# A gated recurrence and two feed-forward stages on one core: the first three levels of the recurrence's pair products in two bursts per block

## The chip, the cores and the metric

The kernel runs on one core of a Trainium2 chip. The metric is device time in microseconds (us) of one execution, as the median of the runs.

## The reference

Three layers in fp32 follow each other. Cut to what matters:

```python
# r, k, v, w: (4, 8, 768, 48)   u: (8, 48)
for t in range(768):
    cur = einsum('bhd,bhe->bhde', u * k[t], v[t])
    y[t] = einsum('bhd,bhde->bhe', r[t], state + cur)
    state = w[t][..., None] * state + einsum('bhd,bhe->bhde', k[t], v[t])
x = y.transpose(0, 2, 1, 3).reshape(3072, 384)
xn = x / sqrt(mean(x * x) + 1e-6) * rms_g
x1 = (silu(xn @ w_gate) * (xn @ w_val)) @ w_out        # 384 -> 1536 -> 384
h = relu(x1 @ w_in)
out = (s * h * h + b) @ w_out2                          # 384 -> 2048 -> 384
```

## The kernel before

**The work.** 3072 tokens are cut into six groups of 512, and each group into two blocks of two chunks of 128 tokens. The attention of group s (called stage s here, s = 0 to 5) is computed while the gated layer of group s-1 runs; the squared layer of all groups follows at the end. A stage of the gated layer has 36 steps k: gate tile, value tile and output tile in turn, each nine wide matmuls (128x128 weights, 512 moving columns; weights and x are each split in an upper and a lower part, three products for one). Between the steps every engine has a fixed list of attention work, in `attention(s, k)` of each engine. The order on an engine is the program's; engines meet by semaphores alone.

**The attention.** The recurrence with its decays is worked out by levels. K and R hold keys and queries by channel (48 channels of a head in 64 rows, two heads on 128 partitions, 8 times 128 tokens in the columns). At level l, tokens stand in runs of 2^l; the products of the first runs' keys with the second runs' queries are what that level gives. After a level the keys of first runs are multiplied by the decay over the second run (VectorE, `multiply_keys`), the queries of second runs by the decay over the first (GpSimd, `multiply_queries`), and the decays themselves are doubled (VectorE, `double_decay`, called by `decays_after`). The products of a level are matmuls of 64 rows, 64 key columns, and 32 moving query columns, 32 of them a block (8 column blocks, two halves, two heads): `level`. They land in `level_ps` (two PSUM banks, shared by both blocks: 16 tiles of 64 columns); VectorE copies what the mask of the level lets through into `near` (`place`, copy_predicated). Level 5 (`NEAR`) is copied by ScalarE (`place_near`), and level 6 by `place_far`.

**Where it is put in.** In a later stage (s > 0) levels 1 to 5 are at steps `LEVEL_AT = (3, 6, 9, 12, 15)`, both blocks in one burst of TensorE, the top level at 18. The keys are turned at 20 (chunks 0 to 2) and 22 (chunk 3), copied by ScalarE (`keys_out`), and multiplied with the values at 22 (`update` 0, 1) and 24 (`update` 2, 3); `attend` follows at 24 and 26. `advance_state` on VectorE adds the updates. At step 34 GpSimd multiplies the next stage's queries for level 0, and VectorE its decays and keys; ScalarE makes x_hi at 33.

**The gated layer on the other engines.** ScalarE makes the silu of the gate tile behind the gate step (L806) and u_hi behind the value step (`upper`, L813); VectorE the product u (`product`, L1057) in the value step and u_lo (`lower`, L1065) in the step after that. TensorE's output tile needs u_lo of its f, its next gate tile the silu, and its next value tile the product. In stage 1 ScalarE and VectorE also split weights (`upper_weights` L785, `upper_out_weights` L790; `lower_weights` L1042, `lower_out_weights` L1047), which the gated layer of the first group needs in turn.

TensorE's waits in a level are these (in the functions below `wait(pe, sem, n)` holds the engine until the count is reached):

```python
elif l > 1:
    level_out(pe, s, l - 1, blk)      # the level before has been placed
if s > 0 and l == 1:
    wait(pe, yo_done, CH * s)
keys_ready(pe, s, l, blk)
queries_ready(pe, s, l, blk)
```

## Time and profile before

| what | value |
|---|---|
| median of 3 runs | 1009.8 us (1008.68 to 1010.35) |
| the profiled execution, its own time | 1010.07 us |
| its span, first to last instruction | 1007.9 us |
| TensorE busy | 990.4 us (98%) |
| VectorE busy | 548.2 us (54%) |
| ScalarE busy | 314.0 us (31%) |
| GpSimd busy | 267.3 us (27%) |
| mean granted TensorE clock | 0.986 of full |

The rows call the engines PE (TensorE's matmuls), PEld (its weight loads), DVE (VectorE), ACT (ScalarE) and POOL (GpSimd). Matmuls overlap, so the distance between starts is what one costs, not its duration. An fp32 matmul of the program is two rows in the trace, of weights and of matmul alike. A bracket at the end of a row is the idle time of the engine ahead of it and what ended it.

### The profile page before, as it was taken

The numbers are of one execution on the slowest core, as the hardware profiler recorded it, in microseconds if no ns is written. First come the engines' busy times: TensorE is split into PE (matmuls) and PEld (weight loads), VectorE is DVE, ScalarE is ACT, GpSimd is POOL, SyncE is SP. The second block draws the span as 40 slices with busy tenths as digits, with TensorE's granted clock in tenths as the row PEclk, the third lists the DMA queues.
The fourth block names the chain that finished last, engine by engine and source line by source line (L and its number), as shares of the span: only waits on it lengthen the run. The fifth ranks groups of instructions, "written<-read, shape, count | busy, mean of one in ns | idle before, by whom it ended". The sixth has DMA issues, their size and how long they took to land.

```text
span 1007.9 us, 24185 instructions
## 1 busy us (share of the span) xinstructions
PE 990.4 (98%) x10344; PEld 830.3 (82%) x10344; DVE 548.2 (54%) x738; ACT 314.0 (31%) x530; POOL 267.3 (27%) x189
## 2 busy tenths in 40 slices
PE   7889999999999999999999999999999999999998
PEld 6778888888888888888888888888888888888898
DVE  6789866764776477557753225506337054162440
ACT  1442323232223313231323445405225043151340
POOL 4655723552464156216610560000000000000000
PEclk7799999999999999999999999999999999999999
DMA  7380252117013601440116201011020110201000
GB/s 272 119 318 15 90 158 101 49 45 224 33 49 106 194 3 49 142 158 2 49 49 207 94 28 64 1 24 40 11 52 0 21 42 10 52 0 21 11 8 24
DMA packets 70780, 74.02 MB, mean 73 GB/s; under 512 B 50464, under 2 KB 55072, under 8 KB 69408
## 3 DMA queue, kind: packets, MB, share of 16 engines
q1 hardware_dynamic: 70112, 71.52, 22.3%
q8 instruction: 75, 1.23, 0.5%
q10 hardware_dynamic: 576, 1.13, 0.3%
q14 instruction: 17, 0.14, 0.0%
HBM read 59.27 MB, written 13.37 MB: 72 GB/s over the span
## 4 chain that ended last, share of the span: by engine, by line
PE 87%; DVE 1%; issue 0%; ACT 0%; DVEq 0%
PE value_o_ps L609 13%; PE mix_gate_ps L609 13%; PE o_ps L1402 11%; PE level_ps L47 10%; PE o_ps L621 9%; PE mix_gate_ps L1402 5%; PE value_o_ps L47 5%; PE mix_gate_ps L47 5%; PE value_o_ps L621 4%; PE level_ps L481 4%; PE o_ps L1415 2%; PE mix_gate_ps L557 2%; PE level_ps L557 2%; PE mix_gate_ps L1415 1%; PE value_o_ps L1415 1%; PE level_ps L535 1%
## 5 line engine op out<-in xcount | busy, mean ns | idle before, releaser
L1189 POOL TENSOR_TENSOR R<-R,arena 128x512 f32<-128x512 f32 x72 | 117.2, 1644 | 187.6 <-PE level_ps L481 169.1
L1501 DVE SCALAR_TENSOR_TENSOR sqr<-relu,sb_col 128x512 f32<-128x512 f32 x96 | 72.3, 753 | 73.1 <-ACT relu L1463 73.1
L1057 DVE TENSOR_TENSOR u_raw<-value_o_ps,u_raw 128x512 f32<-128x512 f32 x66 | 45.5, 690 | 111.6 <-PE value_o_ps L609 111.5
L806 ACT ACTIVATE u_raw<-mix_gate_ps 128x512 f32<-128x512 f32 x72 | 43.0, 598 | 181.1 <-PE mix_gate_ps L609 181.1
L813 ACT ACTIVATE u_hi<-u_raw 128x512 fp32r<-128x512 f32 x66 | 41.7, 632 | 151.3 <-DVE u_raw L1057 151.3
L609 PE MATMUL mix_gate_ps<-x_hi,w_hi 128*128 128x512 f32 x216 | 84.8, 393 | 0.7 <-DVE x_lo L1018 0.7
L609 PE MATMUL value_o_ps<-x_hi,w_hi 128*128 128x512 f32 x216 | 85.2, 394 | 0.0
L609 PE MATMUL value_o_ps<-x_hi,w_lo 128*128 128x512 f32 x216 | 84.2, 390 | 0.0
L609 PE MATMUL value_o_ps<-x_lo,w_hi 128*128 128x512 f32 x216 | 84.2, 390 | 0.0
L609 PE MATMUL mix_gate_ps<-x_lo,w_hi 128*128 128x512 f32 x216 | 84.2, 390 | 0.0
L609 PE MATMUL mix_gate_ps<-x_hi,w_lo 128*128 128x512 f32 x216 | 84.2, 390 | 0.0
L923 DVE TENSOR_TENSOR K<-K,arena 128x512 f32<-128x512 f32 x72 | 71.5, 1006 | 22.3 <-PE level_ps L481 18.0
L1065 DVE TENSOR_TENSOR u_lo<-u_raw,u_hi 128x512 fp32r<-128x512 f32 x66 | 73.0, 1106 | 12.5 <-ACT u_hi L813 12.1
L1506 DVE SCALAR_TENSOR_TENSOR g_lo<-sqr,sb_col,g_hi 128x512 fp32r<-128x512 f32 x96 | 71.6, 746 | 0.8
L1454 ACT ACTIVATE g_hi<-sqr,sb_col 128x512 fp32r<-128x512 f32 x96 | 68.8, 717 | 1.3 <-DVE sqr L1501 1.3
L1463 ACT ACTIVATE relu<-mix_gate_ps 128x512 f32<-128x512 f32 x24 | 14.4, 598 | 171.6 <-PE mix_gate_ps L47 171.6
L1402 PE MATMUL o_ps<-g_hi,wt_lo 128*128 128x512 f32 x160 | 62.3, 390 | 0.0
L1402 PE MATMUL o_ps<-g_lo,wt_hi 128*128 128x512 f32 x160 | 62.3, 389 | 0.0
L1402 PE MATMUL o_ps<-g_hi,wt_hi 128*128 128x512 f32 x160 | 62.3, 389 | 0.0
L1521 DVE STREAM_TRANSPOSE o_sb<-o_ps 128x512 f32<-128x512 f32 x10 | 7.2, 717 | 101.1 <-PE o_ps L1402 101.1
L621 PE MATMUL o_ps<-u_hi,wo_hi 128*128 128x512 f32 x144 | 60.4, 420 | 0.0
L481 PEld LDWEIGHTS level_ps<-R,K 64*64 64x64 f32 (+1 forms) x3392 | 50.2, 133 | 10.2 <-issue 8.8
(204 smaller groups left out, 2318.5 us busy)
## 6 DMA issues: line engine op xcount, KB each, us to landing
kr_nat<-kr SPq DMA_DIRECT2D x10, 1152.0 KB, 5.6
K<-kT SPq DMA_DIRECT2D x12, 512.0 KB, 4.3
arena<-wT SPq DMA_DIRECT2D x12, 512.0 KB, 6.4
R<-rT SPq DMA_DIRECT2D x10, 512.0 KB, 4.2
w_raw<-wgv SPq DMA_DIRECT2D x12, 384.0 KB, 5.8
v_sb<-v SPq DMA_DIRECT2D x12, 384.0 KB, 4.3
x_scratch<-x_sb SPq DMA_DIRECT2D x18, 256.0 KB, 2.3
x_raw<-x_scratch SPq DMA_DIRECT2D x6, 768.0 KB, 4.5
```

Source lines behind the costliest of these rows:

```text
L47: mm = pe.matmul(ps, w[:, cols], x[:, k], start=(k == 0 and w is win_hi and x is x_hi), stop=(k == KT - 1 and w is win_lo))
L481: mm = pe.matmul(level_tile(s, l, blk)[i * SUB:i * SUB + keys, h * Q + q], K[blk][rows, first_key:first_key + keys], halves(R[blk][rows, f ...
L609: mm = pe.matmul(ps[:], w[:, f, j, k], x[:, k], start=(k == 0 and w is w_hi and x is x_hi), stop=(k == KT - 1 and w is w_lo))
L621: mm = pe.matmul(o_ps[j][:], w[:, f, j * P:(j + 1) * P], x[:, f % 2], start=(f == 0 and w is wo_hi and x is u_hi), stop=(f == F1 - 1 and w ...
L923: dve.tensor_tensor(k, k, decay(blk, l, 1), ALU.mult).then_inc(kmul_done, 1)
L1057: dve.tensor_tensor(u[:, f % 2], value_ps[:], u[:, f % 2], ALU.mult).then_inc(u_done, 1)
L1065: dve.tensor_tensor(u_lo[:, f % 2], u[:, f % 2], u_hi[:, f % 2].bitcast(F32), ALU.subtract).then_inc(ulo_done, 1)
L1189: pool.tensor_tensor(q, q, decay(blk, l, 0), ALU.mult).then_inc(rmul_done, 1)
L1402: mm = pe.matmul(o_ps[j], w[:, f, j * P:(j + 1) * P], g[:, f], start=(f == 0 and g is g_hi and w is wt[0]), stop=(f == F2 - 1 and g is g_lo))
L1454: act.activation(g_hi[:, f], sq[f % 2][:], ACT.Identity, bias=sb_col[:, 1:2]).then_inc(ghi_done[0], 1)
L1501: dve.scalar_tensor_tensor(out=sq[f % 2][:], in0=relu[f % 2][:], scalar=sb_col[:, 0:1], in1=relu[f % 2][:], op0=ALU.mult, op1=ALU.mult).th ...
L1506: dve.scalar_tensor_tensor(out=g_lo[:, f], in0=sq[f % 2][:], scalar=sb_col[:, 1:2], in1=g_hi[:, f].bitcast(F32), op0=ALU.add, op1=ALU.subt ...
```

## The change

In the later stages levels 1 to 3 are made differently; stage 0 and levels 4 to 6 keep their form. The queries of the moving side are copied to a place of their own (`moved`, in the room of y and of x_raw), so that one matmul has the columns of more than one level:

- a lower burst per block with 64 moving columns: 32 of level one; 16 with tokens 4 to 7 of every 16 after level one's multiplication, which meet keys 2 and 3; and 16 with the same queries times one more decay (`carry_queries`, GpSimd), which meet keys 0 and 1, not yet multiplied;
- a middle burst per block with 48 moving columns: 16 of level two for tokens 12 to 15, and 32 of level three.

Level two is thus computed in two halves. `moved` is written by ScalarE (`odd_queries`, `second_queries`, `fourth_queries`, `upper_queries`). Between the bursts VectorE multiplies the keys of level one, and then a quarter of the keys by level two's decay (`advance_first`), after the middle burst another quarter (`advance_third`). Placing is in three copies after a lower burst, and two after a middle one, a block at a time, with three masks more. The lower bursts are at steps 3 and 5, the middle ones at 7 and 9. GpSimd's multiplications of levels 1 to 3 wait for ScalarE's copies instead of TensorE's levels. The fourth turn of keys goes to step 20, all four updates and advances of the state to step 22, and updates take 48 of 64 key columns; reads of the state take 48 rows.

```diff
@@ constants
 LEVEL_AT = (3, 6, 9, 12, 15)
+LOWER_AT, MIDDLE_AT = (3, 5), (7, 9)
+SEG = 16
@@ TensorE
+        def joined_levels(s, blk, width):
+            for q in range(Q):
+                for i in range(2):
+                    for h in range(2):
+                        rows = slice(h * SUB, (h + 1) * SUB)
+                        first_key = q * P + i * SUB
+                        mm = pe.matmul(pairs_ps(s, blk)[i * SUB:(i + 1) * SUB, h * Q + q, 0:width],
+                                       K[blk][rows, first_key:first_key + SUB],
+                                       moved[blk][rows, first_key:first_key + width],
+                                       start=True, stop=True, skip_group_check=True)
+            mm.then_inc(level_done, 1)
+
+        def lower_levels(s, blk):
+            if blk == 0:
+                wait(pe, yo_done, CH * s)
+            else:
+                wait(pe, cp_done, placed(s, 1, 0))
+            keys_ready(pe, s, 1, blk)
+            wait(pe, odd_out, turn_no(s, blk))
+            wait(pe, second_out, turn_no(s, blk))
+            wait(pe, carried, turn_no(s, blk))
+            joined_levels(s, blk, SUB)
+
+        def middle_levels(s, blk):
+            if blk == 0:
+                wait(pe, cp_done, placed(s, 1, 1))
+            else:
+                wait(pe, cp_done, placed(s, 2, 0))
+            wait(pe, first_advanced, turn_no(s, blk))
+            wait(pe, fourth_out, turn_no(s, blk))
+            wait(pe, upper_out, turn_no(s, blk))
+            joined_levels(s, blk, 3 * SEG)
...
-                    mm = pe.matmul(sums_ps(s, n)[h * SUB:(h + 1) * SUB, p * D:(p + 1) * D],
-                                   KTr[n][:, p * P + h * SUB:p * P + (h + 1) * SUB], v_sb[blk][:, c, head * D:(head + 1) * D],
+                    mm = pe.matmul(sums_ps(s, n)[h * SUB:h * SUB + D, p * D:(p + 1) * D],
+                                   KTr[n][:, p * P + h * SUB:p * P + h * SUB + D], v_sb[blk][:, c, head * D:(head + 1) * D],
@@ ScalarE
+        def odd_queries(s, blk):
+            ...
+            wait(act, rmul_done, level_no(s, 0, blk))
+            act.activation(moved_columns(blk, 0, HALF, 2), upper_halves(R[blk][:], 1), ACT.Copy).then_inc(odd_out, 1)
+        def second_queries(s, blk):
+            wait(act, rmul_done, level_no(s, 1, blk))
+            act.activation(moved_columns(blk, HALF, HALF + SEG, 4), by_segment(R[blk][:])[:, :, :, 4:8], ACT.Copy).then_inc(second_out, 1)
+        def fourth_queries(s, blk):
+            wait(act, level_done, matched(s, 1, blk))
+            wait(act, rmul_done, level_no(s, 1, blk))
+            act.activation(moved_columns(blk, 0, SEG, 4), by_segment(R[blk][:])[:, :, :, 12:16], ACT.Copy).then_inc(fourth_out, 1)
+        def upper_queries(s, blk):
+            wait(act, level_done, matched(s, 1, blk))
+            wait(act, rmul_done, level_no(s, 2, blk))
+            act.activation(moved_columns(blk, SEG, 3 * SEG, 8), upper_halves(R[blk][:], 3), ACT.Copy).then_inc(upper_out, 1)
...
+            if k == 0:
+                odd_queries(s, 1)
+            if k == 1:
+                second_queries(s, 0)
+            if k == 2:
+                second_queries(s, 1)
+            if k == 4:
+                fourth_queries(s, 0)
+            if k == 6:
+                upper_queries(s, 0)
+                fourth_queries(s, 1)
+            if k == 8:
+                upper_queries(s, 1)
...
+            if k == NEXT_AT and s + 1 < NSB:
+                odd_queries(s + 1, 0)
@@ VectorE
+            if k in LOWER_AT:
+                blk = LOWER_AT.index(k)
+                multiply_keys(s, 1, blk)
+                advance_first(s, blk)
+                place_lower(s, blk)
+            if k in MIDDLE_AT:
+                blk = MIDDLE_AT.index(k)
+                place_middle(s, blk)
+                advance_third(s, blk)
+            if k == MIDDLE_AT[1]:
+                keys_after(s, 3)
+            if k in LEVEL_AT[3:]:
@@ GpSimd
+                elif s > 0 and l == 1:
+                    wait(pool, odd_out, turn_no(s, blk))
+                elif s > 0 and l == 2:
+                    wait(pool, carried, turn_no(s, blk))
+                    wait(pool, second_out, turn_no(s, blk))
+                    wait(pool, fourth_out, turn_no(s, blk))
+                elif s > 0 and l == 3:
+                    wait(pool, upper_out, turn_no(s, blk))
...
+                    carry_queries(s, 0)
+                    carry_queries(s, 1)
                     own_next(2 * s)
```

## Rows read from the trace of the kernel before

**Rows 1.** Windows, stages 1 and 3: PE, PEld, DVE, ACT, POOL busy; PEclk, DMA share, GB/s.

```profile
58.00:154.00 96.00, 94.55 (x1379) 78.39 (x1378) 78.37 (x102) 31.67 (x55) 46.61 (x30) 1.00 0.43 150
...
250.00:346.00 96.00, 95.85 (x1396) 79.57 (x1395) 62.82 (x85) 25.98 (x48) 40.91 (x28) 1.00 0.27 89
```

**Rows 2.** The chain that ended last, one gate step: start, us, what.

```profile
255.88 2.04 PE mix_gate_ps L609 x9
```

**Rows 3.** Groups by shape, TensorE: levels with 64 and 32 weight columns (busy, mean ns).

```profile
L481 PE MATMUL level_ps<-R,K 64*64 64x32 f32 x2752 | 46.4, 223 | 1.2 <-DVE near L940 1.2
...
L481 PE MATMUL level_ps<-R,K 64*32 64x32 f32 x640 | 6.9, 195 | 0.0
```

**Rows 4.** Timeline of TensorE around level one in stage 1: start, us, what.

```profile
68.03 0.39 PE L609 MATMUL value_o_ps<-x_hi,w_lo 128*128 128x512 f32 x1
68.35 2.07 PE L481 MATMUL level_ps<-R,K 64*64 64x32 f32 x128
70.35 0.50 PE L621 MATMUL o_ps<-u_hi,wo_hi 128*128 128x512 f32 x1
70.69 0.39 PE L621 MATMUL o_ps<-u_lo,wo_hi 128*128 128x512 f32 x1
```

**Rows 5.** Timeline of TensorE: the top level, and level five.

```profile
109.37 1.16 PE L499 MATMUL level_ps<-R,K 64*64 64x64 f32 x64
...
293.28 1.35 PE L481 MATMUL level_ps<-R,K 64*32 64x32 f32 x128
```

**Rows 6.** Timeline of TensorE: updates in stages 0 and 3, first rows of attend.

```profile
43.53 2.07 PE L535 MATMUL mix_gate_ps<-v_sb,arena 128*64 128x48 f32 x64
...
317.58 1.14 PE L535 MATMUL level_ps<-v_sb,arena 128*64 128x48 f32 x32
318.65 0.25 PE L557 MATMUL mix_gate_ps<-v_sb,near 64*64 64x48 f32 x1
```

**Rows 7.** Timeline of all engines around level one in stage 3.

```profile
259.57 0.39 PE L609 MATMUL value_o_ps<-x_hi,w_lo 128*128 128x512 f32 x1
...
259.89 2.07 PE L481 MATMUL level_ps<-R,K 64*64 64x32 f32 x128
260.00 0.69 DVE L1057 TENSOR_TENSOR u_raw<-value_o_ps,u_raw 128x512 f32<-128x512 f32 x1 [1.93 <-PE value_o_ps L609]
260.79 0.63 ACT L813 ACTIVATE u_hi<-u_raw 128x512 fp32r<-128x512 f32 x1 [2.23 <-DVE u_raw L1057]
261.19 0.69 DVE L923 TENSOR_TENSOR K<-K,arena 128x512 f32<-128x512 f32 x1 [0.50 <-PE level_ps L481]
261.23 3.55 POOL L1189 TENSOR_TENSOR R<-R,arena 128x512 f32<-128x512 f32 x2 [20.84 <-PE level_ps L481]
...
262.13 1.48 DVE L923 TENSOR_TENSOR K<-K,arena 128x512 f32<-128x512 f32 x1 [0.24 <-PE level_ps L481]
```

**Rows 8.** Timeline: pairs of operations with 256 elements, ScalarE and VectorE.

```profile
248.18 0.73 ACT L818 ACTIVATE u_hi<-u_raw 128x256 fp32r<-128x256 f32 x2 [1.96 <-DVE u_raw L1060]
...
352.91 0.75 DVE L915 TENSOR_TENSOR arena<-arena 128x256 f32<-128x256 f32 x2
```

**Rows 9.** Timeline of VectorE in stage 0: placing level one, then level two.

```profile
15.69 1.30 DVE L940 COPY_PREDICATED near<-masks,o_ps 128x512 f32<-128x512 uint8 x1
...
18.65 0.68 DVE L940 COPY_PREDICATED near<-masks,level_ps 128x512 f32<-128x512 uint8 x1
```

**Rows 10.** Timelines of VectorE and GpSimd in stage 3, at the same time.

```profile
272.88 2.28 DVE L1065 TENSOR_TENSOR u_lo<-u_raw,u_hi 128x512 fp32r<-128x512 f32 x1
...
272.78 1.84 POOL L1203 TENSOR_TENSOR kr_nat<-kr_nat,u_b 128x768 f32<-128x768 f32 x1
```

**Rows 11.** Timelines of VectorE, ScalarE and GpSimd in stage 1.

```profile
69.07 0.95 DVE L1042 TENSOR_TENSOR w_lo<-w_raw,w_hi 128x768 fp32r<-128x768 f32 x1
...
72.32 0.85 ACT L790 ACTIVATE wo_hi<-wo_raw 128x768 fp32r<-128x768 f32 x1
...
62.69 1.51 POOL L1189 TENSOR_TENSOR R<-R,arena 128x512 f32<-128x512 f32 x1 [2.10 <-issue]
```

More of the change, by code:

```diff
@@ L327, in x_quadrants, with by_segment, moved_columns, upper_halves @@
         return x_raw[:].rearrange("p k (a b f) -> p k a b f", a=QUAD, b=2)[:, :, :, blk]
+    def by_segment(ap):
+        return ap.rearrange("p (t g e) -> p t g e", t=2 * Q, e=SEG)
+    def moved_columns(blk, first, last, m):
+        return moved[blk].rearrange("p (t c) -> p t c", c=SUB)[:, :, first:last].rearrange("p t (g m) -> p t g m", m=m)
+    def upper_halves(ap, l):
+        return halves(ap, l)[:, :, 1].rearrange("p (t g) m -> p t g m", t=2 * Q)
     def halves(ap, l):
@@ L468, in level @@
                 level_out(pe, s, l - 2, blk)
-            elif l > 1:
-                level_out(pe, s, l - 1, blk)
-            if s > 0 and l == 1:
-                wait(pe, yo_done, CH * s)
+            else:
+                level_out(pe, s, l - 1, 1)
             keys_ready(pe, s, l, blk)
@@ L512, in turn_keys @@
                 wait(pe, far_done, copied(0, 0))
-            elif n == 3:
+            elif n == 3 and not batch_end(CH * s + 1):
                 wait(pe, kt_out, turned(CH * s) + 1)
@@ L525, in update @@
             blk, c = n // C, n % C
-            wait(pe, kt_out, turned(CH * s + n) + 1)
-            if n % 2 == 0 and not batch_end(CH * s + n + 1):
-                wait(pe, kt_out, turned(CH * s + n + 1) + (1 if n == 0 else 0))
+            if s > 0:
+                wait(pe, kt_out, turned(CH * s + CH))
+            else:
+                wait(pe, kt_out, turned(n) + 1)
+                if n % 2 == 0:
+                    wait(pe, kt_out, turned(n + 1) + (1 if n == 0 else 0))
             wait(pe, far_done, copied(s, 0))
@@ L884, in _ @@
         first_attention()
+        odd_queries(1, 0)
         for s in range(1, NSB + 1):
@@ L921, in multiply_keys @@
                 wait(dve, level_done, matched(s, l, blk))
+            if s > 0 and l == 3:
+                wait(dve, first_advanced, turn_no(s, blk))
             k = halves(K[blk][:], l)[:, :, 0]
@@ new lines, in advance_third, with place_halves @@
+        def advance_third(s, blk):
+            keys_ready(dve, s, 2, blk)
+            decay_ready(dve, s, 2, blk)
+            wait(dve, level_done, matched(s, 2, blk))
+            advance_quarter(s, blk, 2).then_inc(kmul_done, 1)
+        def place_halves(blk, l, src):
+            m = 1 << l
+            mask = masks[:, l].rearrange("p (n m) -> p n m", m=m).unsqueeze(1).broadcast_to([P, 2 * Q, HALF // m, m])
+            return dve.copy_predicated(near[:, :, blk].rearrange("p j (n two m) -> p j n two m", two=2, m=m)[:, :, :, 1], mask,
+                                       src.rearrange("p j (n m) -> p j n m", m=m))
@@ new lines, in place_quarter, with place_lower @@
+        def place_quarter(blk, which, mask, src):
+            dst = near[:, :, blk].rearrange("p j (g e) -> p j g e", e=SEG)[:, :, :, 4 * which:4 * which + 4]
+            mask = mask.rearrange("p (g m) -> p g m", m=4).unsqueeze(1).broadcast_to([P, 2 * Q, SUB // SEG, 4])
+            return dve.copy_predicated(dst, mask, src.rearrange("p j (g m) -> p j g m", m=4))
+        def place_lower(s, blk):
+            wait(dve, y_done, 2 * s)
+            wait(dve, near_done, copied(s - 1, 1))
+            wait(dve, level_done, matched(s, 1, blk))
+            place_halves(blk, 1, pairs_ps(s, blk)[:, :, 0:HALF]).then_inc(cp_done, 1)
+            wait(dve, cp_done, placed(s, 1, blk) - 2)
+            place_quarter(blk, 1, quarter_masks[:, 0], pairs_ps(s, blk)[:, :, HALF:HALF + SEG]).then_inc(cp_done, 1)
+            wait(dve, cp_done, placed(s, 1, blk) - 1)
+            place_quarter(blk, 1, quarter_masks[:, 1], pairs_ps(s, blk)[:, :, HALF + SEG:SUB]).then_inc(cp_done, 1)
@@ L943, in sum_alpha, with place_middle @@
+        def place_middle(s, blk):
+            wait(dve, cp_done, placed(s, 1, 1))
+            wait(dve, level_done, matched(s, 2, blk))
+            place_quarter(blk, 3, quarter_masks[:, 2], pairs_ps(s, blk)[:, :, 0:SEG]).then_inc(cp_done, 1)
+            wait(dve, cp_done, placed(s, 2, blk) - 1)
+            place_halves(blk, 3, pairs_ps(s, blk)[:, :, SEG:3 * SEG]).then_inc(cp_done, 1)
         def sum_alpha(b):
```

71 lines of the change are left out of this document (56 added, 15 removed).

## The prediction

> **What bounds the kernel now.** I read the page's busy shares first, then the windows by stage, then the timeline around the level bursts. TensorE is busy 990.4 of 1007.9 us, and in two windows of 96 us, one per later stage, it is busy 95.85 of 96.00 at full granted clock (2.4 GHz), while in stage 1 it is busy 94.55; VectorE is busy 78.4 us in stage 1 and 62.8 in stage 3, ScalarE 26 to 32, GpSimd 41 to 47 [rows 1]. Nothing holds TensorE: a saved microsecond of its work is a microsecond gained, and a new wait of it is lost in full. A step k of a stage is nine wide matmuls in 2.04 us [rows 2]; work for the next stage's attention is put in as bursts between steps. So there are two questions: how much TensorE work goes away, and whether the other three engines are still in time for the burst.
>
> **TensorE's work, levels one to three.** A program's fp32 matmul is two rows of the trace: 32 matmuls of one block are 64 rows. A burst of both blocks is 128 rows, started 0.32 us after the last wide matmul started, 2.07 us long including the 0.22 that one row lasts: (2.07-0.22)/127 = 14.6 ns each [rows 3, 4]. From the last wide matmul before it to the second after it is 2.66 us instead of 2 x 0.227, so the burst costs 2.21: 1.86 for its rows and 0.35 for getting in and out [rows 4]. Three such bursts go (384 rows, 5.59 us a stage). Four of 64 rows come. What does a row with 64 moving columns cost? The top level has it, same tile, same weights: (1.16-0.22)/63 = 14.9 ns [rows 5]. So moving columns up to 64 are nearly free; what counts is the weights, because level five with 32 weight columns takes (1.35-0.2)/127 = 9.1 ns [rows 3, 5]. New levels: 256 x 14.9 = 3.81 us. Saved 1.78 a stage, 8.9 us over five stages. The fourth burst's own 0.35 us gives back 1.7. Bounds for a row of 64 columns: 14.6 and, if moving columns set the price, twice that (a rival below); the nearest row says 14.9 and I take it.
>
> **Updates and merges.** Updates are 256 rows in the later stages and 64 in stage 0, at (2.07-0.22)/63 = 29.4 ns, with two tiles side by side, so 59 ns per tile [rows 6]. Per tile of four the level rows give 58 ns with 64 weight columns and 36 with 32, a straight line puts 48 at 47: 11 ns less per tile, 5.5 per row, 320 rows, 1.8 us saved. Bounds: nothing (a 48 is handled as a 64), and 2.4 (a quarter of 29.4). The Trainium skill (TensorE: Matmul & The Clock Gate, section LDWEIGHTS) lets a weight load go as its columns over 1.2, thus 13.3 ns less per tile, by which the term would be an estimated 2.1 us. Putting the last two updates beside the first two leaves out one change from update to attend, 318.65-317.58 less 32 x 0.0294, that is 0.13 us, five times at most: 0.5 [rows 6]. The fourth turn of keys in step 20 must wait for the first copy out in one stage only (3), some 0.2 us; nothing for it. **Sum of TensorE's work: -8.9+1.7-1.8-0.5 = -9.5 us.**
>
> **The new hand-offs.** Before, one pair of key multiplications and one placement for both blocks followed a burst, and the next burst was three steps away. Now lower burst 0 is at step 3, lower 1 at 5, middle 0 at 7, middle 1 at 9; both blocks share the PSUM tile, so each waits until the previous one has been placed. Two steps are all there is. Let X be the start of a lower burst. It holds 64 rows: the first wide matmul after it starts at X+1.07, the second 0.34 later, two steps end so that the next burst could start at X+5.36 (1.07+0.34+16x0.227+0.32).
>
> VectorE's chain behind it: its first key multiplication starts at X+1.30 (261.19-259.89) [rows 7], takes 0.69; then waits of 0.04 for its own results, the advance of a quarter with 256 elements 0.42 (a pair takes 0.75 [rows 8]), the placing of level one with 512 elements 1.29 (the row with runs of two elements, against 0.68 for runs of four [rows 9]; it follows without a wait, 0.09 overlapped), and two quarters of 256 elements, 0.42 each by 0.68 less half of the elements. X+1.30+0.69+0.04+0.42-0.09+1.29+0.04+0.42+0.04+0.42 = X+4.57, and TensorE starts 0.10 later: 0.7 us before X+5.36.
>
> Burst lower 1: does that 0.7 last? GpSimd enters. Its level-two multiplication of block 0 no longer waits for the level burst but for fourth_queries on ScalarE, which starts behind the u_hi copy (1.22 to 1.85 after the last wide matmul, [rows 7]) and takes 0.41 (a pair of 256 elements takes 0.73 [rows 8]): GpSimd begins 2.2 to 2.3 after that matmul, VectorE's advance would at 2.35. The rows show that a multiplication of VectorE that meets one of GpSimd stands until it has ended: the second K multiplication takes 1.48 instead of 0.69, and u_lo 2.28, ending 0.54 after GpSimd's 1.84 [rows 7, 10]. GpSimd's takes 1.5 [rows 11], so the advance is 1.4 late, less 0.7 of slack: **0.7 us of wait**. Bounds: 0 if VectorE comes first, 0.9 with the 1.59 that u_lo lost, 2.2 if two GpSimd operations go first. The Trainium skill (GPSIMD Engine Reference, section Key points) says that GpSimd shares its SBUF interfaces with VectorE, in contention where a VectorE instruction has two SBUF inputs. By that rule the advances and K multiplications suffer, and the placings, with their source in PSUM, don't; the trace agrees (u_raw from PSUM keeps 0.69).
>
> Burst middle 0: it needs upper_queries of block 0, which stands on ScalarE behind u_hi of step 6, which stands behind the product u of step 6, and that on VectorE behind the whole placing of lower 1. The product starts at X+4.48 instead of X+3.4, ends X+5.17; ScalarE 0.10 later, 0.63 for u_hi, then upper_queries of 512 elements, 0.63 less 0.11 overlap, X+6.42; TensorE X+6.5 against X+5.36: **1.15 us of wait**. Bounds: 0.4 (if the three placings take two thirds) and 2 (one GpSimd operation in the way; none is due, since it waits for fourth_queries of block 1, which comes later). Middle 1 at step 9 and level four at step 12: upper_queries of block 1 follows the gate of step 8 and is there a microsecond ahead; the keys of level three come about 2 us ahead. No wait. So too at steps 0 to 3 of stages 2 to 5: odd_queries at step 34 falls where ScalarE has nothing, the rest fits between steps 0 and 2, GpSimd works a chain it formerly idled through (20.84 us idle [rows 7]). Stages 2 to 5: 4 x (0.7+1.15) = 7.4 us.
>
> Stage 1 is tighter. GpSimd's level-zero multiplication ends only at 64.2 [rows 11]; two of level one and the first carry (256 elements, about 0.8) make 68.0 with no contention, while lower 0 wants to start at 68.35 [rows 4]. VectorE has the keys of level zero, wo_lo, u_lo and decays in that time, all with two SBUF inputs: two collisions of 0.6 put lower 0 0.8 late, and w_lo, needed at step 5, about 0.7. Lower 1 0.7 as above. At middle 0 a w_lo (0.95 less 0.09 of overlap) stands before the product and a wo_hi (0.85 less 0.10) before upper_queries [rows 11]: 1.15+0.86+0.75 = 2.8. Stage 1: 5.0 us (2 to 9).
>
> **Sum.** The profiled execution took 1010.07 us (span 1007.9 and 2.2 around it). 1010.07-9.5+7.4+5.0 = 1013.0; it was 0.3 above the median of 1009.8, so 1012.7.
>
> **Rivals.**
> 1. *The hand-offs fit* (other side). VectorE's advance gets in before GpSimd, and stage 1 keeps pace. What decides is lower 1 starting at X+5.36 and middle 0 under 0.6 late. For it: 0.7 us of slack without contention, a race of 0.1 us. Against: the order on ScalarE. 4 x 0.6 + 1.5 = 3.9 of waits: -5.6, 1004 us.
> 2. *Only middle 0 waits, stage 1 costs 3*: -9.5+4.6+3 = -2, about 1008.
> 3. *GpSimd starves VectorE*. Its new chain and own_next run back to back; two operations ahead of the advance (2.2), middle 0 at 1.5, stage 1 at 8: -9.5+14.8+8 = +13; with half of that excess +8, 1018.
> 4. *Moving columns set the price*: 64 columns 29 ns, 48 columns 22: new levels 6.5 us a stage instead of 3.8, +13.6 on top. The top level's row speaks plainly against it.
>
> **How the numbers follow.** Forecast 0.45 (its own range 1008.5 to 1016.5), rival 1 0.25, rival 2 0.12, rival 3 0.15, rival 4 0.03. A measurement here tells 0.2%, 2 us. Faster: rival 1's 0.25, half of 2, and 0.01 of the forecast: 0.32. Same: half of 2 and the forecast's lower part of 0.17: 0.23. Slower: 0.27 of the forecast, 3 and 4: 0.45. The range of 8 in 10 takes in rival 1's middle and rival 3's: 1003 to 1019.
>
> **What would show it.** In the trace of the changed kernel: rows of 64 moving columns near 14.9 ns, four bursts of about 1.0 us each a stage; update rows near 24 ns; waits of TensorE in front of the second and third of the four bursts, released by VectorE's placing and by ScalarE's copy of the upper queries, 1.15 us and the same in every stage; a quarter advance of 1.5 to 2 us beside a GpSimd row; waits in stage 1 above 3 us together. Wrong if TensorE stays busy 95.8 of 96 (then it is rival 1), or if a burst of 64 rows takes over 1.3 us.

## The result, and the profile after

The changed kernel takes 1012.89 us (median of 12 runs, 1012.02 to 1015.95) against 1010.15 of the kernel before (median of 12 runs beside it): 1.0031 times as long, 95% interval 1.0023 to 1.0039. The prediction was 1012.7 and slower, which is 2.9 us above the 1009.8 that it started from; the measured difference is 2.7. Its total is right; two of its terms are not, and their errors nearly cancel. That the total came out so close is luck.

The page of the changed kernel, span and busy time of each engine:

```profile
span 1010.4 us, 23059 instructions
PE 984.3 (97%) x9704; PEld 821.0 (81%) x9704; DVE 551.8 (55%) x783; ACT 330.9 (33%) x570; POOL 272.5 (27%) x199
```

TensorE is busy 6.1 us less than before, and the span is 2.5 us longer. So work went and idle time came. (Busy time is no exact measure of the work saved: a matmul at half the clock counts for longer.) The windows of the same stretches as [rows 1], and one of 2 us in stage 1:

```profile
58.00:154.00 96.00, 89.08 (x1220) 72.50 (x1220) 78.47 (x105) 32.48 (x57) 46.42 (x32) 0.98 0.36 131
250.00:346.00 96.00, 94.68 (x1271) 77.76 (x1270) 63.58 (x93) 29.93 (x56) 41.56 (x30) 1.00 0.28 92
86.00:88.00 2.00, 2.00 (x6) 1.52 (x6) 2.00 (x3) 0.00 (x0) 2.00 (x2) 0.50 0.00 0
```

Stage 3 has 1.17 us of idle time more than before (95.85 less 94.68), stage 1 5.5 more. The third row is the one to stop at: in stage 1 TensorE ran at a granted clock of 0.50, that is 1.2 GHz, where the kernel before has 1.00 throughout this stage. The waits of TensorE in stages 1 to 5, with their sum, number and longest:

```profile
PE level_ps L524 <- ACT y L848: 7.4, 5, 2.7
PE mix_gate_ps L676 <- DVE w_lo L1200: 1.5, 1, 1.5
PE mix_gate_ps L624 <- DVE state L1157: 1.1, 1, 1.1
PE level_ps L524 <- DVE near L1082: 0.8, 1, 0.8
PE o_ps L688 <- DVE u_lo L1223: 0.5, 1, 0.5
```

Five waits for ScalarE's copy of the upper queries, one a stage; but the wait for the placing of the lower burst, which was predicted five times, is there once. The other four rows are all of stage 1. Bursts and updates in the timeline of TensorE, stage 0 and stage 3:

```profile
41.34 1.64 PE L602 MATMUL mix_gate_ps<-v_sb,arena 128*48 128x48 f32 x64
...
264.41 1.16 PE L524 MATMUL level_ps<-y,K 64*64 64x64 f32 x64
...
269.81 1.16 PE L524 MATMUL level_ps<-x_raw,K 64*64 64x64 f32 x64
...
276.45 1.15 PE L524 MATMUL level_ps<-y,K 64*64 64x48 f32 x64 [1.17 <-ACT y L848]
```

A row with 64 moving columns costs (1.16-0.22)/63 = 14.9 ns, as predicted; 264.41 to 269.81 is 5.40 us, the pace of two steps with a burst (5.36 predicted); 269.81 to 276.45 is 6.64, so the middle burst is 1.24 late by its start.

**Where the time went.** To place it, take the first silu of each stage in the timeline of ScalarE (its L902, formerly L806): 61.13, 163.59, 258.40, 354.12, 449.01 us; before 62.34, 158.39, 253.88, 350.26, 445.67. The first silu behind stage 5 is at 543.81 and was at 541.29. Changed less before is -1.21, +5.20, +4.52, +3.86, +3.34 and +2.52. So stage 1 is **6.41 us longer**, each of stages 2 to 5 is 0.5 to 0.8 **shorter** (2.68 together), and stage 0 ends 1.21 earlier: -1.21+6.41-2.68 = +2.52.

Of the 1.21 the updates explain 0.4. The rest is no gain to count on: in the repeat of the changed kernel (experiment 9) stage 1 begins at 64.65, 3.5 us later than here. One difference at this place shows in every profile. All twelve of kernels with the new updates, the changed kernel's among them, have a stretch at 1.2 GHz at the turn from stage 0 to stage 1, somewhere between 55 and 63 us; the one profile of the kernel before has none. The same window, changed and before:

```profile
56.00:58.00 2.00, 2.00 (x12) 2.00 (x11) 1.14 (x3) 1.57 (x4) 1.30 (x1) 0.50 0.90 330
56.00:58.00 2.00, 1.17 (x9) 0.94 (x10) 1.39 (x4) 0.33 (x1) 0.79 (x2) 1.00 0.99 385
```

What it costs and why it comes, no run here settles.

Stage 1 in the timeline of TensorE, the rows with a wait or a burst, and one of the slow stretch:

```profile
67.14 1.16 PE L524 MATMUL level_ps<-y,K 64*64 64x64 f32 x64
68.85 0.50 PE L688 MATMUL o_ps<-u_hi,wo_hi 128*128 128x512 f32 x1 [0.54 <-DVE u_lo L1223]
...
72.73 0.47 PE L676 MATMUL mix_gate_ps<-x_hi,w_hi 128*128 128x512 f32 x1 [1.54 <-DVE w_lo L1200]
...
75.88 1.16 PE L524 MATMUL level_ps<-x_raw,K 64*64 64x64 f32 x64 [0.83 <-DVE near L1082]
...
84.12 1.15 PE L524 MATMUL level_ps<-y,K 64*64 64x48 f32 x64 [2.73 <-ACT y L848]
...
87.04 0.63 PE L676 MATMUL mix_gate_ps<-x_hi,w_lo 128*128 128x512 f32 x1
...
91.12 1.15 PE L524 MATMUL level_ps<-x_raw,K 64*64 64x48 f32 x64
```

The starts of the bursts are 8.74, 8.24 and 7.00 us apart where 5.40 would do: 3.34, 2.84 and 1.60 lost, 7.8 together. The first two are waits (an idle time in brackets is some 0.1 less than what the start moves, since two matmuls overlap). The last one has no wait: eight wide matmuls between 85.78 and 89.17 come 0.42 us apart instead of 0.227, at half the clock, 8 x 0.2 = 1.6. Not all of it is the clock's to give back. Experiments 4 and 10 have the same levels in stage 1 and the full clock there, and in both TensorE comes to the output step behind the last of the four bursts before its wo_lo is there, and waits 0.96 and 0.97 us for it (experiment 1 shows why). Against a stage at full clock the slow stretch costs about 0.6.

### The profile page after: what moved, and what is told of

The parts are those of the page before. It is cut to its first block, busy times and chain, and to the rows that moved or that the text cites. A ratio compares the mean times of both kernels' runs of the same rounds, so it can differ in the third digit from the quotient of the medians.

```text
span 1010.4 us, 23059 instructions
## 1 busy us (share of the span) xinstructions
PE 984.3 (97%) x9704; PEld 821.0 (81%) x9704; DVE 551.8 (55%) x783; ACT 330.9 (33%) x570; POOL 272.5 (27%) x199
## 3 DMA queue, kind: packets, MB, share of 16 engines
q8 instruction: 70, 1.15, 0.5%
## 4 chain that ended last, share of the span: by engine, by line
PE 84%; DVE 2%; issue 1%; ACT 0%; DVEq 0%; ACTq 0%
PE mix_gate_ps L676 13%; PE value_o_ps L676 12%; PE o_ps L1588 11%; PE level_ps L47 10%; PE o_ps L688 9%; PE mix_gate_ps L1588 5%; PE value_o_ps L47 5%; PE mix_gate_ps L47 5%; PE value_o_ps L688 4%; PE level_ps L524 2%; PE o_ps L1601 2%; PE mix_gate_ps L624 2%; PE level_ps L624 2%; PE level_ps L511 1%; PE mix_gate_ps L1601 1%; PE value_o_ps L1601 1%
## 5 line engine op out<-in xcount | busy, mean ns | idle before, releaser
L1366 POOL TENSOR_TENSOR R<-R,arena 128x512 f32<-128x512 f32 x72 | 112.8, 1577 | 187.4 <-PE level_ps L511 62.5
L902 ACT ACTIVATE u_raw<-mix_gate_ps 128x512 f32<-128x512 f32 x72 | 43.1, 598 | 165.3 <-PE mix_gate_ps L676 165.3
L1223 DVE TENSOR_TENSOR u_lo<-u_raw,u_hi 128x512 fp32r<-128x512 f32 x66 | 64.4, 976 | 15.9 <-ACT u_hi L909 15.9
L1036 DVE TENSOR_TENSOR K<-K,arena 128x512 f32<-128x512 f32 x62 | 52.5, 865 | 16.2 <-PE level_ps L511 7.9
L688 PE MATMUL o_ps<-u_hi,wo_lo 128*128 128x512 f32 x144 | 56.4, 392 | 0.0
```

The lines of the kernel that those rows point to most:

```text
L688: mm = pe.matmul(o_ps[j][:], w[:, f, j * P:(j + 1) * P], x[:, f % 2], start=(f == 0 and w is wo_hi and x is u_hi), stop=(f == F1 - 1 and w ...
L902: act.activation(u[:, f % 2], gate_ps[:], ACT.Silu).then_inc(silu_done, 1)
L1036: dve.tensor_tensor(k, k, decay(blk, l, 1), ALU.mult).then_inc(kmul_done, 1)
L1223: dve.tensor_tensor(u_lo[:, f % 2], u[:, f % 2], u_hi[:, f % 2].bitcast(F32), ALU.subtract).then_inc(ulo_done, 1)
L1366: pool.tensor_tensor(q, q, decay(blk, l, 0), ALU.mult).then_inc(rmul_done, 1)
```

## The experiments

The runs were made on three occasions, each beside its own runs of the kernel before (medians 1010.17, 1009.65 and 1010.46), so ratios are compared, and stretches within the traces. Each run has one profile. Stage lengths are taken from first silu to first silu, as above.

**1. The upper queries a step earlier.** `upper_queries` of block 0 stands on ScalarE behind the u_hi copy of step 6. It does not need it.

```diff
-            if k == 6:
+            if k == 5:
                 upper_queries(s, 0)
+            if k == 6:
                 fourth_queries(s, 1)
```

> The changed kernel with one call moved: upper_queries of block 0 is issued at step 5, behind the gate's silu, instead of step 6 behind u_hi; nothing else. Theory A (the wait of 1.17 us in front of the first middle burst is the place in ScalarE's order, behind product u and u_hi): the waits on ScalarE go in all five stages (7.4 us in the profile of the changed kernel: 4 x 1.17 and 2.7), nothing takes their place in stages 2 to 5, since the placing ends 0.7 us ahead; about 1005.5 us, 0.9955 of the kernel before. Theory B (the four bursts two steps apart are too close as such: VectorE's placing and GpSimd are next and hold the burst as well): the wait stays at over half, released by VectorE, and the time stays above 1009.

1010.91 us, ratio 1.0007 (0.9999 to 1.0016): 2 us better than the changed kernel, and not the 1005.5 that was expected. Yet in stages 2 to 5 the wait is gone, and each stage is 1.67, 1.87, 1.72 and 2.06 us shorter than before; the window of stage 3 and one of stage 1:

```profile
250.00:346.00 96.00, 95.85 (x1276) 78.75 (x1275) 65.85 (x94) 30.35 (x56) 41.66 (x30) 1.00 0.29 95
...
96.00:100.00 4.00, 4.00 (x11) 3.13 (x10) 4.00 (x9) 0.06 (x1) 0.00 (x0) 0.50 0.00 0
```

This gives the saved work by itself: 7.3 us in four stages, 1.8 a stage, against the 1.9 of the prediction's -9.5. And it shows the middle wait to be what the prediction said, a copy behind a u_hi that is late, since moving the copy alone removes it. Stage 1 however is 8.55 us longer than before, instead of 6.41. Timelines of TensorE, VectorE and GpSimd there:

```profile
94.88 0.76 PE L688 MATMUL o_ps<-u_hi,wo_hi 128*128 128x512 f32 x1 [4.72 <-DVE wo_lo L1206]
...
87.55 2.93 DVE L1027 TENSOR_TENSOR arena<-arena 128x64 f32<-128x64 f32 x2
90.40 1.86 DVE L1201 TENSOR_TENSOR w_lo<-w_raw,w_hi 128x768 fp32r<-128x768 f32 x1
92.18 2.55 DVE L1206 TENSOR_TENSOR wo_lo<-wo_raw,wo_hi 128x768 fp32r<-128x768 f32 x1
...
86.18 1.16 POOL L1367 TENSOR_TENSOR R<-R,arena 128x512 f32<-128x512 f32 x1 [8.45 <-ACT x_raw L843]
87.30 2.03 POOL L1388 TENSOR_TENSOR kr_nat<-kr_nat,u_b 128x768 f32<-128x768 f32 x1
89.29 2.16 POOL L1367 TENSOR_TENSOR R<-R,arena 128x512 f32<-128x512 f32 x2
91.40 2.52 POOL L1392 TENSOR_TENSOR kr_nat<-kr_nat 128x768 f32<-128x768 f32 x1
```

A wait of 4.72 us for wo_lo takes the place of the one removed. GpSimd runs from 86.18 to 93.92 without a break. Beside it two decays of VectorE (one row, 1.25 in the changed kernel) take 2.93 together, and its two splits, 0.94 us each elsewhere, take 1.86 and 2.55; the splits end at 92.26 and 94.73, both 0.8 after a row of GpSimd has ended (91.45 and 93.92), as if each had waited for it and then run. Rival 3 of the prediction thus exists, in this one place.

Why is GpSimd's chain closed here and not in the changed kernel? Its first row is released in both by the same copy (L843), which was not moved. The difference is a break later on. GpSimd and VectorE in stage 1 of the changed kernel, and GpSimd, VectorE and TensorE in that of experiment 4, where the clock stays full:

```profile
91.01 1.10 POOL L1366 TENSOR_TENSOR R<-R,arena 128x512 f32<-128x512 f32 x1 [2.38 <-ACT x_raw L848]
89.64 0.94 DVE L1205 TENSOR_TENSOR wo_lo<-wo_raw,wo_hi 128x768 fp32r<-128x768 f32 x1
...
91.91 1.12 POOL L1366 TENSOR_TENSOR R<-R,arena 128x512 f32<-128x512 f32 x1 [0.93 <-ACT x_raw L848]
91.99 1.86 DVE L1205 TENSOR_TENSOR wo_lo<-wo_raw,wo_hi 128x768 fp32r<-128x768 f32 x1
94.00 0.47 PE L688 MATMUL o_ps<-u_hi,wo_hi 128*128 128x512 f32 x1 [0.96 <-DVE wo_lo L1205]
```

The multiplication of the second block for level three waits for ScalarE's copy of that block's upper queries, and that copy stands behind the silu of step 8, so behind the late middle burst. In the changed kernel GpSimd stands still for 2.38 us, and both splits run in the gap at 0.94 us. At full clock the silu is earlier and the gap 0.93: wo_lo takes 1.86 and TensorE waits 0.96. In experiment 1, without the wait in front of the burst, there is no gap. So the removed wait had been hiding GpSimd's work. The clock adds to it: from 94.88 to 100.14 twelve wide matmuls run at half the clock, about 2.4 us lost.

**2. GpSimd's `own_next` a burst later.** The predicted 0.7 us at the second lower burst did not come. The theory: VectorE won its race against GpSimd by 0.46 us, because u_lo was held up earlier, by `own_next`, and that held up the product, u_hi and GpSimd's release, but not VectorE's advance.

```diff
-                    own_next(2 * s)
                 if l == 2:
+                    own_next(2 * s)
                     own_keys(2 * s)
```

> The changed kernel with GpSimd's own_next of the even block moved from behind the carried queries to behind the level-two multiplications of queries. Theory A (a VectorE operation with two SBUF inputs stands while a GpSimd operation runs; own_next at the end of the chain delays u_lo and so product u at step 3): u_lo of step 2 in stages 2 to 5 shrinks from 2.3 us to 0.7 to 1.5, the product comes 0.6 us earlier, GpSimd's level-two multiplication starts earlier and now meets the first advance, which rises from 0.42 to 1.5 us or more and makes the second lower burst wait up to 0.7 us: stages 2 to 5 lose 0 to 2.8 us in sum. In stage 1 the w_lo wait (1.54) and u_lo wait (0.54) shrink by about 1.5 together. In sum 1011.5 to 1014.5 us. Theory B (no such blocking; VectorE in stage 1 simply has too much to do): u_lo keeps 2.3 us, nothing moves, 1012.9.

1014.60 us, 1.0052 (1.0036 to 1.0069), just above the 1011.5 to 1014.5 expected. VectorE and GpSimd in stage 3 of the changed kernel:

```profile
262.80 2.33 DVE L1223 TENSOR_TENSOR u_lo<-u_raw,u_hi 128x512 fp32r<-128x512 f32 x1
265.05 0.68 DVE L1215 TENSOR_TENSOR u_raw<-value_o_ps,u_raw 128x512 f32<-128x512 f32 x1
265.74 0.69 DVE L1036 TENSOR_TENSOR K<-K,arena 128x512 f32<-128x512 f32 x1
266.47 0.43 DVE L1060 TENSOR_TENSOR K<-K,arena 128x256 f32<-128x256 f32 x1
266.81 1.30 DVE L1076 COPY_PREDICATED near<-masks,level_ps 128x512 f32<-128x512 uint8 x1
...
262.56 2.02 POOL L1377 TENSOR_TENSOR kr_nat<-kr_nat 128x768 f32<-128x768 f32 x1
266.93 1.16 POOL L1366 TENSOR_TENSOR R<-R,arena 128x512 f32<-128x512 f32 x1 [2.35 <-ACT y L843]
```

and with `own_next` later (VectorE, GpSimd, TensorE, then the row of its waits):

```profile
263.34 0.68 DVE L1223 TENSOR_TENSOR u_lo<-u_raw,u_hi 128x512 fp32r<-128x512 f32 x1
...
267.01 1.39 DVE L1060 TENSOR_TENSOR K<-K,arena 128x256 f32<-128x256 f32 x1
...
266.96 1.16 POOL L1366 TENSOR_TENSOR R<-R,arena 128x512 f32<-128x512 f32 x1 [3.83 <-ACT y L843]
...
270.63 1.16 PE L524 MATMUL level_ps<-x_raw,K 64*64 64x64 f32 x64 [0.20 <-DVE near L1082]
...
PE level_ps L524 <- DVE near L1082: 1.6, 5, 0.8
```

In the changed kernel u_lo takes 2.33 us and the advance (L1060) 0.43. Without `own_next` there, u_lo takes 0.68, GpSimd starts 0.05 before the advance instead of 0.46 behind it, the advance takes 1.39, and the lower burst waits 0.20 us, five times in all instead of once. So the race that the prediction described is real and is lost when nothing else is late. The predicted price was too high: 0.2 us, since the advance takes 0.96 longer and not 1.4. GpSimd's multiplication lasts 1.16 us there and not the 1.5 that was taken for it, and it had begun before. The placing (L1076), which reads PSUM, takes 1.30 us from 266.81 in the changed kernel, with GpSimd busy from 266.93 to 268.09 beside it, and 1.29 with none beside it in the other. In stage 1 the wait for w_lo went, and one of 1.4 for a wo_lo came. Stages 2 to 5 are 0.3 us longer each than in the changed kernel, 1.2 together; the rest of the 1.7 between the medians is not placed.

**3. The old levels, the new updates.** The updates, the turn of keys and the joined step 22 alone, with levels 1 to 3 as before. Against the changed kernel, TensorE's lines (the other engines' are left out):

```diff
-            if k in LOWER_AT:
-                lower_levels(s, LOWER_AT.index(k))
-            if k in MIDDLE_AT:
-                middle_levels(s, MIDDLE_AT.index(k))
-            if k in LEVEL_AT[3:]:
+            if k in LEVEL_AT:
```

> The kernel before with the change's second part alone: updates with 48 key columns, reads of the state with 48 rows, the fourth turn of keys at step 20, all updates at step 22; levels 1 to 3 as before. By the prediction's sum 1.8+0.5 = 2.3 us less than before; by the rows of the changed kernel (updates (1.28-0.21)/47 = 22.8 ns a row instead of 29.4, 320 rows: 2.1; and 0.5) 2.6 us less: 1007.5 us, 0.9975. The rival, that the moved advances of the state hold attend in stage 1 as in the changed kernel (1.1 us there), gives 1008.6. If the levels' part alone is what costs, this one is faster by more than 0.2%.

1008.74 us, 0.9986 (0.9977 to 0.9995), the figure of the rival in the expectation. Stages 2 to 5 are 0.49, 0.52, 0.47 and 0.62 us shorter than before, stage 1 only 0.08. There is a wait in stage 1 that the prediction did not have, and that stands here without the new levels:

```profile
PE mix_gate_ps L560 <- DVE state L1009: 1.0, 1, 1.0
```

`attend` waits for the state, which VectorE advances among weights that it still has to split (step 21 has a wo_lo). In the kernel before the same wait was 0.6. It varies from profile to profile: 1.1 in the first one of the changed kernel, 0.3 in its repeat.

**4. Updates with 64 columns again**, all else as changed.

```diff
-                    mm = pe.matmul(sums_ps(s, n)[h * SUB:h * SUB + D, p * D:(p + 1) * D],
-                                   KTr[n][:, p * P + h * SUB:p * P + h * SUB + D], ...
+                    mm = pe.matmul(sums_ps(s, n)[h * SUB:(h + 1) * SUB, p * D:(p + 1) * D],
+                                   KTr[n][:, p * P + h * SUB:p * P + (h + 1) * SUB], ...
```

> The changed kernel with updates of 64 key columns again, all else as changed. By the rows 2.1 us more TensorE work (29.4 instead of 22.8 ns for 320 rows), nothing hides it: 1015.0 us, 1.0050 of before. If 48 columns were worth nothing, 1012.9.

1014.93 us, 1.0044 (1.0031 to 1.0058): 2.0 above the changed kernel's median, 1.3 by the ratios. 1015.0 was expected. Stages 2 to 4 are 0.33, 0.21 and 0.18 us shorter than before where the changed kernel has 0.68, 0.66 and 0.52: 0.38 a stage for 64 rows. The update rows of stage 3:

```profile
318.73 2.07 PE L602 MATMUL level_ps<-v_sb,arena 128*64 128x48 f32 x64
```

against 1.64 and 1.65 for 64 rows of 48 columns: (1.64-0.2)/63 = 22.8 ns a row and 29.4. That is 6.6 ns a row, 13.2 a tile, and 320 rows make 2.1 us. The prediction took 1.8. The Trainium skill (TensorE: Matmul & The Clock Gate, section LDWEIGHTS) has a weight load take its columns over 1.2 in ns, an estimated 13.3 ns for 16 columns less per tile; the trace agrees with 13.2.

**5. Experiment 1 for stages 2 to 5 alone.** If the loss of experiment 1 lies in stage 1, leaving stage 1 as it was in the changed kernel should bring both results together.

```diff
-            if k == 5:
+            if s > 1 and k == 5:
                 upper_queries(s, 0)
             if k == 6:
+                if s == 1:
+                    upper_queries(s, 0)
```

> As e1, but stage 1 keeps the changed kernel's order (upper_queries of block 0 behind u_hi of step 6 where s is 1, at step 5 from stage 2 on). Theory A (the order on ScalarE costs 1.17 us in each of stages 2 to 5, as e1's trace has it; in stage 1 e1's earlier release lets five operations of GpSimd run in a row, and VectorE's decays, w_lo and wo_lo stand behind them): the 4.7 us wait for wo_lo of e1 is absent, the 1.17 us waits of stages 2 to 5 too: 1012.9 - 4.7 = 1008.2 us, 0.998 of before. Theory B (e1's loss in stage 1 was an accident of its weights' arrival): the wo_lo wait comes again in some size, 1010 to 1011.

1008.58 us, 0.9984 (0.9975 to 0.9993), against 1008.2 expected: faster than before by 0.16%. Stage 1 is 6.4 us longer than before, as in the changed kernel, the others 1.7 to 2.1 shorter each. The wait of 4.72 us is gone, and GpSimd's gap in stage 1 is back with 2.42 us.

**6. Stage 1 as before, stages 2 to 5 as in experiment 1.**

```diff
-            if k in LOWER_AT:
+            if s > 1 and k in LOWER_AT:
                 lower_levels(s, LOWER_AT.index(k))
-            if k in MIDDLE_AT:
+            if s > 1 and k in MIDDLE_AT:
                 middle_levels(s, MIDDLE_AT.index(k))
-            if k in LEVEL_AT[3:]:
+            if k in (LEVEL_AT if s == 1 else LEVEL_AT[3:]):
...
-            if k == 6:
+            if s > 1 and k == 5:
                 upper_queries(s, 0)
...
```

(`...` stands for lines left out here; the other engines take the new form from stage 2 on in the same way)

> Stage 1 with levels 1 to 3 of the kernel before (bursts of 128 rows at 3, 6, 9), stages 2 to 5 with the new levels and upper_queries at step 5; updates as changed. If the only faults are stage 1 and the order on ScalarE, the stages' differences add: stages 2 to 5 by e1's trace 1.67+1.87+1.72+2.04 = 7.3 us less than before, stage 1 as in e3 (0.1 less), stage 0's updates 0.4: 1002.4 us, 0.9923 of before. If something else in the new levels costs, over 1005.

1002.28 us, 0.9930 (0.9916 to 0.9944), with 1002.4 expected. Stage 1 is now as long as before (-0.05), and the four other stages 1.5 to 1.9 us shorter each. The change pays in stages 2 to 5; stage 1 spends it.

**7. Experiment 6, and the wo_lo of step 21 moved to step 25**, for the wait for the state.

```diff
-LATE_OUT = (8, 13, 16, 21, 27)
+LATE_OUT = (8, 13, 16, 25, 27)
```

> e6 with the fifth wo_lo of stage 1 (0.95 us, 1.51 with a GpSimd operation in the way) moved on VectorE from step 21 to 25; TensorE needs it at step 28. Theory: the wait of 1.0 us of attend for the advanced state in stage 1, seen in the changed kernel, e1, e2 and e3 alike, comes from VectorE being late at step 22 with four advances in a row; it goes: 1.0 us less than e6, 1001.4. Rival: the advances wait for the updates, not for VectorE, then nothing moves.

1001.33 us, 0.9918 (0.9904 to 0.9931), the best version of all. The wait for the state is gone; of the waits in levels this one is left:

```profile
PE level_ps L530 <- DVE near L1084: 0.2, 1, 0.2
```

In stage 3 its four bursts start at 258.97, 264.37, 269.77 and 275.16: 5.40 apart, at the pace of TensorE. Against experiment 6 the gain of 1.0 is within what two medians of five runs tell apart; the wait that went was 1.0, and stage 1 is 0.9 shorter than there.

**8. Experiment 1 with less beside it in stage 1.** GpSimd's `own_*` of the even block of stage 1 is cut to 16 of its 768 elements, so this kernel leaves out the rest of these products.

```diff
-            pool.tensor_tensor(kr_nat[:, 2], kr_nat[:, 2], kr_nat[:, 0], ALU.mult).then_inc(next_done, 1)
+            n = 16 if b == 2 else C * DM
+            pool.tensor_tensor(kr_nat[:, 2, 0:n], kr_nat[:, 2, 0:n], kr_nat[:, 0, 0:n], ALU.mult).then_inc(next_done, 1)
```

(and the same in `own_keys` and `own_products`)

> e1 with the three operations of GpSimd on the own keys of stage 1's even block (own_next, own_keys, own_products) cut to 16 of 768 elements, so the rest of those products is left out; order and waits are unchanged. Theory A (VectorE's two-input operations stand behind GpSimd's): VectorE's decays, w_lo and wo_lo in steps 7 and 8 of stage 1, 2.93, 1.86 and 2.55 us in e1, fall to about 1.5, 0.95 and 0.95 or little over, the wait for wo_lo falls from 4.7 us to under 2, the time by 3 to 5: about 1006.5. Theory B (VectorE simply has too much work of its own there): its rows keep their length, 1010.5.

1004.89 us, 0.9958 (0.9943 to 0.9973). The same operations of VectorE as in experiment 1, and TensorE's wait:

```profile
84.90 1.31 DVE L1027 TENSOR_TENSOR arena<-arena 128x64 f32<-128x64 f32 x2
86.14 0.94 DVE L1201 TENSOR_TENSOR w_lo<-w_raw,w_hi 128x768 fp32r<-128x768 f32 x1
87.01 1.85 DVE L1206 TENSOR_TENSOR wo_lo<-wo_raw,wo_hi 128x768 fp32r<-128x768 f32 x1
...
89.00 0.47 PE L688 MATMUL o_ps<-u_hi,wo_hi 128*128 128x512 f32 x1 [1.53 <-DVE wo_lo L1206]
```

2.93, 1.86 and 2.55 became 1.31, 0.94 and 1.85, and the wait 1.53 instead of 4.72, though VectorE's own work is the same. The rival that VectorE simply has too much of its own is thus out. The last split fell less than expected (0.95): a multiplication of GpSimd from 86.34 to 88.03 still stands beside it. The time is 1.6 us under the 1006.5 expected, since stage 1 also ran at full clock. Of the 6.6 us that it is shorter than in experiment 1, 3.2 are this wait, 0.9 the wait for u_lo at step 4 (1.46 to 0.58) and some 2.4 the clock (single profiles: that of experiment 1 is of the slowest of its twelve runs, this one of the fastest of its four).

**9. The changed kernel again**, as the control for 10 and 11.

> The changed kernel once more, on the chip of e9 and e10, to compare them on one chip: 1.003 of before, waits and clock in stage 1 as before: 2.7 us at the middle burst, 1.5 for w_lo, a stretch of 3.4 us at half clock in stage 1.

1014.80 us, 1.0044 (1.0030 to 1.0059), the same waits as at first (2.7, 1.5, 0.8, 0.5), but 0.3 instead of 1.1 for the state, and again a stretch at 1.2 GHz. Stage 1 is 5.80 us longer than before, where the first profile has 6.41.

**10. One w_lo from step 5 to 6**, out of the chain ahead of the middle burst of stage 1.

```diff
-LATE_WEIGHTS = (5, 7, 9, 11, 14, 17, 20, 23, 28)
+LATE_WEIGHTS = (6, 7, 9, 11, 14, 17, 20, 23, 28)
```

> The changed kernel with one w_lo of stage 1 moved on VectorE from step 5 to step 6, behind product u (TensorE needs it at step 8). The prediction split stage 1's wait at the first middle burst into 1.15 (the order), 0.86 (this w_lo) and 0.75 (a wo_hi on ScalarE). Theory A: 2.7 falls by 0.86 to 1.9, the rest as it was: 0.9 us less in all, a little more if the half clock goes with it. Theory B (VectorE's work is only shifted and u_lo or the placing is late instead): a wait of the same size elsewhere, no change.

1012.36 us, 1.0018 (1.0008 to 1.0027). The middle wait fell from 2.75 to 1.88, the w_lo's own share of the prediction's sum, as theory A has it. Other waits came: 2.0 for u_lo at step 4, where the control has 1.5 for w_lo and 0.5 for u_lo, and 1.0 for wo_lo. In sum TensorE's waits in stage 1 are 6.1 us, against 5.9 in the control. And still stage 1 is 1.65 us shorter than in the control. Windows of both from 80 to 154 us, the control first:

```profile
80.00:154.00 74.00, 70.83 (x1060) 58.12 (x1051) 61.74 (x81) 20.96 (x37) 33.71 (x24) 0.98 0.23 75
```

```profile
80.00:154.00 74.00, 70.66 (x1032) 58.16 (x1031) 61.65 (x79) 21.59 (x38) 34.54 (x24) 1.00 0.26 82
```

The granted clock is 1.00 instead of 0.98: the stretch of 3.4 us at half clock, worth 1.6, is not there. The wait for wo_lo belongs to that and not to the moved w_lo, since experiment 4 has it too, with w_lo in its old place and the clock full. Nor is the longer wait for u_lo its doing: it comes at step 4, ahead of the place that w_lo left, and experiment 1 has it too (1.46, and none for w_lo). So of the 1.65 us 0.9 are the middle wait, and 0.6 the clock's 1.6 less the 1.0 for wo_lo. Theory B is not borne out. The profiled execution was the fastest of ten (1011.02), so whether the others kept the full clock is not known.

**11. The changed kernel with the `own_*` of experiment 8 cut.**

> The changed kernel with own_next, own_keys and own_products of stage 1's even block cut to 16 of 768 elements (the rest of these products is left out), as in e8. What GpSimd's blocking costs stage 1 in the changed kernel itself: the w_lo wait of 1.54 us at step 5 falls by 1.0 to 1.5, as own_next (2.3 us at 68.2) no longer stands in front of the decays; the middle burst's 2.7 stays, since no such operation is between the second lower burst and it. 1 to 2 us less than the changed kernel. If VectorE's own load is the cause, nothing changes.

1012.42 us, 1.0018 (1.0006 to 1.0030). This is 2.4 below the control's median, more than the 1 to 2 expected; stage 1 is 0.84 shorter. The waits for u_lo and w_lo in steps 4 and 5, 1.5 to 2.2 together in experiments 1, 4, 5 and 10 and the control, are 0.7 (0.6 in experiments 2 and 8, which take `own_next` away from there too), and the 2.7 ahead of the middle burst stays. So the first came largely from GpSimd's work beside VectorE's and the second did not. The stretch at half clock stays too.

## Why the prediction was right, and where it was not

- **TensorE's work, -9.5: right.** Rows with 64 moving columns cost 14.9 ns. The updates saved 2.1 instead of 1.8 (experiment 4). Experiment 1, all but without waits in stages 2 to 5, has them 1.8 shorter each.
- **Middle burst 0 waits 1.15 a stage: right**, in place, releaser and size (1.17 of idle time, 1.24 by starts). The chain behind the lower burst at X = 269.81 was predicted as product at X+4.48, burst at X+6.5; it came at X+4.58 (274.39) and X+6.64. Experiment 1 shows the cause in stages 2 to 5 by removing it.
- **Lower burst 1 waits 0.7 in stages 2 to 5: wrong, it waits 0.** The step that failed is "GpSimd begins 2.2 to 2.3 after that matmul, VectorE's advance would at 2.35". Measured from that matmul, at 264.09, the advance does start at 2.38, but GpSimd only at 2.84. The prediction took the product to start on time. It starts behind u_lo, which stands beside `own_next`: the product ran at 265.05, 0.64 after the start of the lower burst, where it was 0.11 after it in [rows 7], and only what hangs on it moved. The prediction had the rule (a VectorE multiplication stands until GpSimd's has ended) and applied it to the advance alone, not to the one u_lo that decides who comes first. Experiment 2 turns the race round, with 0.2 us for its price. 4 x 0.7 = 2.8 too much. Rival 2 ("only middle 0 waits") is what stages 2 to 5 did.
- **Stage 1 costs 5.0: too low, 8.3 in this profile.** Worked out as 7.8 for the three distances above and 0.5 for the state (1.1 less 0.6). By parts: the lower burst 0, w_lo and lower burst 1 had 2.2 and measured 3.34, the middle one had 2.8 and measured 2.84; experiment 10 takes out its w_lo share alone (0.9), while the share of wo_hi (0.75) was not tested by itself. The rest are two terms that the prediction did not have, 0.5 for the state (which the repeat does not show) and 1.6 for the clock, of which 1.0 would have come as a wait for wo_lo at full clock, a hand-off that the prediction did not have either. 3.3 too little. With the saved work, 8.3-1.9 = 6.4, what stage 1 is longer.
- **The sum.** -2.8 and +3.3 cancel to 0.5 us; that is luck and not insight. What came is the waits of rival 2 in stages 2 to 5 with a stage 1 near the top of the forecast's own 2 to 9 us, and none of the listed cases put these two together. Rival 1 was right that VectorE's advance comes before GpSimd and wrong about the middle burst and stage 1, rival 3 about how often (GpSimd starves VectorE only in stage 1, where VectorE also has weights to split), and rival 4 about the price of moving columns.

The Trainium skill (GPSIMD Engine Reference, section Key points) has a VectorE instruction with two SBUF inputs contend with GpSimd. Experiments 1, 2 and 8 agree: such instructions stretch from 0.94 to 2.55 and from 0.43 to 1.39 us beside GpSimd and shrink again when it is taken away (w_lo from 1.86 to 0.94, wo_lo to 1.85), and placings from PSUM don't. The row that the prediction gave for PSUM, 0.69 us at 260.00 in [rows 7], has no GpSimd row beside it, so it shows nothing of this; the placing of 1.30 and 1.29 us in experiment 2 does.

What stays open is why the granted clock fell in stage 1. In the profiles of the changed kernel and its repeat, and of experiments 1, 2, 5 and 11, a stretch at 1.2 GHz follows TensorE's idle times there; in those of 3, 6, 7 and 8, which have fewer, there is none. But there is none in those of 4 and 10 either, whose waits in stage 1 add up to 7.4 and 6.1 us (of which 1.0 comes only behind the place of the stretch), while experiment 11 has the stretch with 5.5. Idle time came first each time; why it was followed by the low clock in the one and not in the other, these runs don't settle, and a single profile of each doesn't tell how often it is. The same holds for the stretch at the turn from stage 0 to stage 1.

## What to carry to other kernels

Before a hand-off on a tight engine is moved closer, walk the chain behind it on the other engines, and put each of their delays on everything that follows, not only on the instruction in question: who wins a race of half a microsecond was decided two instructions earlier. A stage that also prepares weights is another kernel than the steady ones; price it by itself, and give it the old form if it can't carry the new one: that, with one copy and one split moved, turned 0.3% slower into 0.8% faster here. When a removed wait brings less than its length, look for what it had been hiding: here a gap in GpSimd's chain, in which VectorE got its weights split in time, was there only because TensorE was late.
